# Gated linear attention before a mixture of experts: the attention output formed in 32-row array tiles, turned by VectorE instead of TensorE, and the state decay moved to ScalarE

## What is computed

```python
# q, k, v, alpha: (4, 8, 768, 48)
for t in range(S):
    state = alpha[:, :, t, :, None] * state + np.einsum('bhd,bhe->bhde', k[:, :, t], v[:, :, t])
    y[:, :, t] = np.einsum('bhd,bhde->bhe', q[:, :, t], state)
x = y.transpose(0, 2, 1, 3).reshape(3072, 384)
p = domain_probs / (domain_probs.sum(-1, keepdims=True) + 1e-09)
x2 = sum(p[:, e:e + 1] * (np.maximum(x @ w1[e], 0.0) @ w2[e]) for e in range(4))   # w1 (4, 384, 1024)
h = x2 @ w_in                                                                      # (384, 2048)
out = (h * np.clip(h + 3.0, 0.0, 6.0) / 6.0) @ w_out
```

## Time and profile before

| | |
|---|---|
| median of 3 runs | 1420.34 us (1420.33 to 1421.3) |
| the profiled execution | 1419.88 us |
| its span in the trace | 1418.1 us |
| mean granted TensorE clock | 0.996 |
| busy share PE, PEld, DVE, ACT, POOL | 98%, 80%, 52%, 38%, 59% |

### The profile page before, as it was taken

The page is one execution under the profiler, slowest core; times in us unless marked ns, Lnnn a source line. Parts: engine busy times, 40 slices in busy tenths (PEclk is TensorE's granted clock), DMA queues, the critical chain, the costliest instruction groups (busy, mean ns, idle before and its releaser), DMA issues.

```text
span 1418.1 us, 30461 instructions
## 1 busy us (share of the span) xinstructions
PE 1388.5 (98%) x11672; PEld 1140.5 (80%) x11672; DVE 731.3 (52%) x1383; ACT 533.6 (38%) x927; POOL 837.6 (59%) x870
## 2 busy tenths in 40 slices
PE   6789999999999999999999999999999999999998
PEld 5678888888888888888888888888888888888887
DVE  6977665545554555455545455555455343333343
ACT  2133333333344333344433335433334443335553
POOL 8867776565666565656665656565655444444442
PEclk9899999999999999999999999999999999999999
DMA  4333333333333433334333333443332333233330
GB/s 142 119 120 108 102 110 96 106 93 115 93 104 124 138 93 107 93 109 128 107 115 116 93 107 93 136 123 107 93 93 82 113 118 100 90 100 92 99 123 34
DMA packets 70366, 150.10 MB, mean 106 GB/s; under 512 B 9296, under 2 KB 21840, under 8 KB 70224
## 3 DMA queue, kind: packets, MB, share of 16 engines
q1 hardware_dynamic: 70224, 148.16, 34.5%
HBM read 143.36 MB, written 4.77 MB: 104 GB/s over the span
## 4 chain that ended last, share of the span: by engine, by line
PE 93%; POOL 4%; issue 1%; DVE 1%; ACT 0%; DMA 0%; DVEq 0%; POOLq 0%; ACTq 0%
PE h_bank L446 41%; PE out_banks L462 28%; PE out_third L462 14%; PE score_banks L358 4%; POOL k_lev L828 2%; PE score_banks L420 2%; PE turn_bank L398 1%; POOL decay L802 1%; PE score_banks L414 1%; PE turn_bank L386 1%; PE turn_bank L388 1%; POOL w_lo L842 1%; PE turn_bank L374 1%; POOL k_lev L818 0%; DMA alpha_q<-qa 0%
## 5 line engine op out<-in xcount | busy, mean ns | idle before, releaser
L842 POOL TENSOR_TENSOR w_lo<-w_raw,w_hi 128x768 fp32r<-128x768 f32 x288 | 547.6, 1902 | 528.2 <-ACT w_hi L745 528.0
L739 ACT ACTIVATE h_hi<-gated 128x512 fp32r<-128x512 f32 x288 | 182.2, 633 | 670.5 <-DVE gated L590 582.3
L446 PE MATMUL h_bank<-x_hi,w_hi 128*128 128x512 f32 x864 | 336.4, 389 | 1.1 <-issue 1.1
L446 PE MATMUL h_bank<-x_lo,w_hi 128*128 128x512 f32 x864 | 336.1, 389 | 0.0
L446 PE MATMUL h_bank<-x_hi,w_lo 128*128 128x512 f32 x864 | 336.0, 389 | 0.0
L590 DVE SCALAR_TENSOR_TENSOR gated<-h_bank,probs 128x512 f32<-128x512 f32 x192 | 132.7, 691 | 328.0 <-PE h_bank L446 328.0
L604 DVE TENSOR_TENSOR h_lo<-gated,h_hi 128x512 fp32r<-128x512 f32 x288 | 241.6, 839 | 57.5 <-ACT h_hi L739 57.5
L745 ACT ACTIVATE w_hi<-w_raw 128x768 fp32r<-128x768 f32 x288 | 239.1, 830 | 8.0 <-DMA w_raw<-w 8.0
L462 PE MATMUL out_banks<-h_hi,w_hi 128*128 128x512 f32 x576 | 233.0, 405 | 0.3 <-DVE x_lo L614 0.3
L462 PE MATMUL out_banks<-h_hi,w_lo 128*128 128x512 f32 x576 | 225.0, 391 | 0.0
L462 PE MATMUL out_banks<-h_lo,w_hi 128*128 128x512 f32 x576 | 224.5, 390 | 0.0
(11 more groups left out here) (75 smaller groups left out, 1279.5 us busy)
## 6 DMA issues: line engine op xcount, KB each, us to landing
w_raw<-w SPq DMA_DIRECT2D x288, 384.0 KB, 3.1
alpha_q<-qa SPq DMA_DIRECT2D x48, 256.0 KB, 3.5
k_raw<-kk SPq DMA_DIRECT2D x48, 128.0 KB, 3.5
probs<-prob_scratch SPq DMA_DIRECT2D x6, 1024.0 KB, 7.5
v_diag<-v SPq DMA_DIRECT2D x96, 48.0 KB, 2.4
out<-result SPq DMA_DIRECT2D x18, 256.0 KB, 3.9
level_sb<-level SPq DMA_DIRECT2D x1, 80.0 KB, 3.1
ident_sb<-ident SPq DMA_DIRECT2D x1, 64.0 KB, 2.8
```

The costliest lines, as they stand in the source:

```text
L446: mm = pe.matmul(h_bank[g % 2][:, :], a, x, start=k == 0 and i == 0, stop=k == K3 - 1 and i == 2)
L739: act.activation(h_hi[:, g % DEEP, :], gated[:, g % 2, :], ACT.Copy).then_inc(hh_made, 1)
L842: pool.tensor_tensor(w_lo[:, g % RING, :], w_raw[:, g % RAW, :], w_hi[:, g % RING, :].bitcast(F32), ALU.subtract).then_inc(w_lo_made, 1)
```

## The change

- `attend(n)` writes each output into a quarter of the partitions. `quarter(i, jp)` is 32 partitions, 64i+32jp. The 64 steps of a chunk are two halves `th`; half `th` is 32 columns of weights. L414 becomes 8 matmuls (16 instructions) on tiles of 128 rows by 32 columns, still 96 values moving; L420 becomes 16 matmuls (32 instructions) on tiles of 64 rows by 32 columns, 48 values moving.
- `copy_y` on ACT and `turn_y` on TensorE are gone. A new `turn_y(n)` on DVE turns 32x32 blocks straight from PSUM to SBUF (`y_turned`), two instructions of 64 partitions by 192 elements, right behind `next_state(n)`. The order of channels that comes out differs, so the host orders the rows of `w1` to match.
- `split_x` reads `y_turned` in SBUF instead of PSUM, on ACT and on DVE, one slot after the state slot. `TURN_AT` is gone. The bank (now `state_bank`) holds `kv_out` and `kt_out` alone, and the waits of `turn_k` and `carry` on `x_hi_made` and `x_lo_made` go.
- `decay_state(n)` moves from DVE (one instruction) to ACT, four instructions of 128x48 with `total` as scale, in the slot after the score slot, in the prologue after `copy_k_rows(n)`.

The core of the diff (declarations, semaphore names and the host's index arithmetic left out):

```diff
@@ tensor engine @@
             def score(n):
-                need(pe, ys_made, 2 * (n - 1) if n <= PER_TILE else 2 * n)
+                need(pe, yt_made, 2 * (n - 1) if n <= PER_TILE else 2 * n)
...
             def turn_k(n):
                 need(pe, s_made, carried(n))
-                need(pe, x_hi_made, n - 1)
-                need(pe, x_lo_made, n - 1)
-                if n % PER_TILE == 0:
-                    need(pe, x_hi_made, n)
-                    need(pe, x_lo_made, n)
...
-            def turn_y(n):
-                pe.wait_ge(ys_made, 2 * (n + 1))
-                need(pe, s_made, carried(n + 1))
-                need(pe, x_hi_made, n)
-                need(pe, x_lo_made, n)
-                rows = y_rows[n % 2]
-                for i in range(2):
-                    pe.matmul(turn_bank[own(i), P:P + CH], rows[:, P:STATE], ident_sb[:, own(i)],
-                              start=True, stop=True)
-                pe.transpose(turn_bank[:, 0:P], rows[:, 0:P], ident_sb[:, :]).then_inc(xt_made, 1)
...
             def attend(n):
-                for jp in range(2):
-                    for i in range(2):
-                        lo = 512 * i + jp * 2 * HEAD_D
-                        mm = pe.matmul(y_out[own(i), lo:lo + 2 * HEAD_D], p_kept[:, i, jp, :],
-                                       v_diag[n % 2][:, :, jp, i, :], start=jp == 0, stop=not inter,
-                                       skip_group_check=True)
-                for j in range(PAIRS if inter else 0):
-                    for i in range(2):
-                        lo = 512 * i + j * HEAD_D
-                        mm = pe.matmul(y_out[own(i), lo:lo + HEAD_D], q_level(n, LEVELS)[own(i), j, :],
-                                       state[n % 2][own(i), j, :], start=False, stop=True,
-                                       skip_group_check=True)
+                for th in range(2):
+                    for jp in range(2):
+                        for i in range(2):
+                            lo = 512 * i + th * 2 * HEAD_D
+                            mm = pe.matmul(y_out[quarter(i, jp), lo:lo + 2 * HEAD_D],
+                                           p_kept[:, i, jp, 32 * th:32 * th + 32], v_diag[n % 2][:, :, jp, i, :],
+                                           start=th == 0, stop=not inter, skip_group_check=True)
+                for th in range(2 if inter else 0):
+                    for jj in range(2):
+                        for jp in range(2):
+                            for i in range(2):
+                                j, lo = 2 * jp + jj, 512 * i + (2 * th + jj) * HEAD_D
+                                mm = pe.matmul(y_out[quarter(i, jp), lo:lo + HEAD_D],
+                                               q_level(n, LEVELS)[own(i), j, 32 * th:32 * th + 32],
+                                               state[n % 2][own(i), j, :], start=False, stop=True,
+                                               skip_group_check=True)
...
@@ vector engine @@
-            def decay_state(n):
-                dve.tensor_tensor(state_decayed[:, :, :], state[n % 2][:, :, :], ...
+            def turn_y(n):
+                dve.wait_ge(y_made, n + 1)
+                need(dve, x_hi_made, n - 1)
+                need(dve, x_lo_made, n - 1)
+                for i in range(2):
+                    dve.transpose(y_turned[n % 2][own(i), :, :].rearrange("p b (h t) -> p h b t", t=32),
+                                  scores(n)[own(i), 512 * i:512 * i + STATE].rearrange(
+                                      "p (h b e) -> p h b e", h=2, e=32)).then_inc(yt_made, 1)
...
                 if g - 1 in SCORE_AT:
-                    n = SCORE_AT[g - 1]
-                    if n % PER_TILE > 0:
-                        split_x(n - 1)
-                    keep_all(n, 3, KEEPS)
-                    if not first_of_seq(n) and not last_of_seq(n):
-                        decay_state(n)
+                    keep_all(SCORE_AT[g - 1], 3, KEEPS)
+                if g - 1 in STATE_AT:
+                    split_x(STATE_AT[g - 1])
...
+                if g in STATE_AT:
+                    n = STATE_AT[g]
+                    if not last_of_seq(n):
+                        next_state(n)
+                    turn_y(n)
@@ scalar engine @@
-            def copy_y(n):
-                for i in range(2):
-                    act.activation(y_rows[n % 2][own(i), :], scores(n)[own(i), 512 * i:512 * i + STATE], ACT.Copy
+            def decay_state(n):
+                act.wait_ge(s_made, carried(n))
+                act.wait_ge(z_made, Z_STEPS * (n + 1))
+                for j in range(PAIRS):
+                    act.activation(state_decayed[:, j, :], state[n % 2][:, j, :], ACT.Copy,
+                                   scale=total[n % 2][:, j:j + 1]).then_inc(dec_made, 1)
```

More of the change, by code:

```diff
@@ L86 @@
 STATE_AT = {state_slot(n): n for n in range(PER_TILE, CHUNKS)}
-TURN_AT = {score_slot(n) + (4 if n < 2 * PER_TILE else 5): n for n in range(2 * PER_TILE - 1, CHUNKS, PER_TILE)}
 def spread(share):
@@ L476, in _ @@
                 keep_warm(2)
-                turn_y(n)
                 if n + 1 < PER_TILE:
@@ L577, in split_x @@
                 dve.wait_ge(x_hi_made, n + 1)
-                if (n + 1) % PER_TILE and not last_of_seq(n + 1):
-                    dve.wait_ge(kn_made, carried(n + 1) + 1)
-                dve.tensor_tensor(x_lo[:, r, :, cols], kv_out.rearrange("p (k t) -> p k t", t=CH),
+                dve.tensor_tensor(x_lo[:, r, :, cols], y_turned[n % 2][:, :, :],
                                   x_hi[:, r, :, cols].bitcast(F32), ALU.subtract).then_inc(x_lo_made, 1)
@@ L671, in _ @@
                 if g - 1 in SCORE_AT:
-                    n = SCORE_AT[g - 1]
-                    if n % PER_TILE > 0:
-                        split_x(n - 1)
-                    keep_all(n, 3, KEEPS)
-                    if not first_of_seq(n) and not last_of_seq(n):
-                        decay_state(n)
+                    keep_all(SCORE_AT[g - 1], 3, KEEPS)
+                if g - 1 in STATE_AT:
+                    split_x(STATE_AT[g - 1])
                 if g in SCORE_AT:
                     keep_all(SCORE_AT[g], 0, 3)
-                if g in STATE_AT and not last_of_seq(STATE_AT[g]):
-                    next_state(STATE_AT[g])
-                if g in TURN_AT:
-                    split_x(TURN_AT[g])
+                if g in STATE_AT:
+                    n = STATE_AT[g]
+                    if not last_of_seq(n):
+                        next_state(n)
+                    turn_y(n)
                 if g in Q_AT:
@@ L759, in _ @@
             for n in range(PER_TILE):
-                if n > 0:
-                    split_x(n - 1)
                 copy_k_rows(n)
+                if not first_of_seq(n):
+                    decay_state(n)
                 odd_k(n + 2)
-                copy_y(n)
-            split_x(PER_TILE - 1)
+                split_x(n)
             for g in range(SLOTS):
@@ L779, in _ @@
                         odd_k(n + 2)
-                if g in STATE_AT:
-                    copy_y(STATE_AT[g])
-                if g in TURN_AT:
-                    split_x(TURN_AT[g])
+                if g - 1 in SCORE_AT:
+                    n = SCORE_AT[g - 1]
+                    if not first_of_seq(n) and not last_of_seq(n):
+                        decay_state(n)
+                if g - 1 in STATE_AT:
+                    split_x(STATE_AT[g - 1])
                 if g >= BEHIND and g - BEHIND + 1 in STARTS and PHASES[PHASE_OF[g - BEHIND]][0] == "E":
@@ L899 @@
     dm, ft = H * D, 8
-    f = np.arange(pairs * D)
-    row = [(2 * (f // D) + i) * D + f % D for i in range(2)]
-    order = np.concatenate([row[0][:P], row[1][:P], row[0][P:], row[1][P:]])
+    b, i, jp, f = np.ix_(range(dm // P), range(2), range(2), range(32))
+    jj, e = np.divmod(32 * b + f, D)
+    order = ((2 * (2 * jp + jj) + i) * D + e).reshape(-1)
     def pack(w1, w2):
```

40 lines of the change are left out of this document (11 added, 29 removed).

## The result

Before 1420.34 us (13 runs), after **1423.28 us** (1421.24 to 1425.02, 13 runs): ratio 1.002, 95% interval 1.0011 to 1.0028. The forecast was 1405.0 us in 1398 to 1415. The change costs 2 to 4 us; it was to give 15.

A forecast was written before the change was run, and what follows sets the result against it. Past the prologue TensorE's own order of work bounds the kernel, in the prologue DVE. Terms -16.1 + 3.6 - 1.3 - 1.5 = -15.3 us take 1420.34 to 1405.0 us, range 1398 to 1415.

The forecast's parts named there:

- The step that failed: DVE, main part: two transposes add 0.6 us, L557's 0.35 goes per chunk, `split_x` moves earlier; no cost.
- The prologue: DVE's rounds lose 0.90 us of decay and gain 0.6 of transposes; six rounds give -1.5 us, bounds -3 and +10.
- DVE paces it, with POOL just behind: Prologue: DVE's rounds follow every 7.17 us without idle time; POOL waits 0.29 us in each for `decay_state`.
- turns: Turn matmuls leave TensorE: 13.3 us from 35 score slots and 2.8 from 5 turn-only slots, together -16.1 us.
- the wait in slot 3: `score(9)` waits for DVE's earlier `turn_y(8)` instead of ACT's copy: -1.3 us, 0 if DVE is as late.
- The narrower tiles: TensorE's `attend`: L414 stays 0.33 us, L420 falls to 0.55, one more shape change costs 0.15; +3.6 us, bounds -6 and +6.
- TensorE waiting for DVE at `score`: A sign in the profile after that would show the prediction wrong; no size given.
- ACT: Gains four 128x48 decays, at most 1.3 us, and loses two L713 of 0.32: net 0.65 per chunk, fits its idle time.
- Narrow tiles that do not overlap: Rival in `attend`: L414 takes 0.66 us and L420 1.07, +36 us in all, giving 1437 us; chance 0.07.
- starts as the floor: Rival in `attend`: 48 starts at 23 ns each take 1.12 us, so no change, 1420 us; chance 0.04.
- Transposes of 1.0 us: Rival on DVE: slow transposes make the prologue cost 8.8 us instead of -1.5, giving 1415 us; chance 0.07.
- idle time of PE behind slot 0: Main part: the profile after was to show none of it; no size given.

The follow-up runs named there:

- experiment 2: Changed kernel with DVE's `split_x` one slot later in the main part, two slots behind the state slot, ACT's unmoved: 1407.71 us, ratio 0.9911 to the kernel before.
- 6: On the kernel with DVE's later `split_x`: prologue `turn_y` moved to the end of DVE's round, behind the last `scale_q` steps; 1409.0 us, ratio 0.9921.
- 9: On the kernel with DVE's later `split_x`: the prologue's `x_lo` subtraction of chunks 0 to 5 on POOL instead of DVE; 1407.48 us, ratio 0.9911.
- 3: Changed kernel with `decay_state` back on DVE as one instruction, in prologue and main part, nothing on ACT: 1426.01 us, ratio 1.0035 to the kernel before.
- 1: Changed kernel with ACT's prologue `odd_k(n+2)` moved ahead of `copy_k_rows(n)` and `decay_state(n)`: 1424.86 us, ratio 1.0034 to the kernel before.
- 7: On the kernel with DVE's later `split_x`: ACT's prologue `odd_k` one chunk further ahead; 1410.32 us, ratio 0.9931.
- 8: On the kernel with DVE's later `split_x`: six idle matmuls instead of two at three `keep_warm` places per prologue chunk; 1407.95 us, ratio 0.9917.
- 11: On the kernel with DVE's later `split_x`: prologue forms one `x_lo` column and turns one 32x32 block in place of six; 1404.81 us, one execution.
- 12: On the kernel with DVE's later `split_x`: prologue forms one `x_lo` column per chunk, all block transposes done; 1409.46 us, one execution.

## Why the prediction was wrong

**The step that failed** is "In the main part DVE adds 0.6 and loses L557's some 0.35 per chunk, beside 328 us of waiting for TensorE: no cost", with "`split_x` moves from the next score slot to the slot behind the state slot". It saw that the result would be ready early and took early for harmless. It named what is queued behind `turn_y`, and never did so for `split_x`. Moved there, DVE stood for 1.7 to 2.2 us for an `x_hi` that ACT makes later in the same slot, with `keep` and the next `hidden_lo` behind it. And that the second operand went from PSUM to SBUF was not costed: 0.35 became 1.61 us, since POOL's `w_lo` runs at that moment. The idle 328 us were a sum over the span; in nine slots, five of them in tile 1, there was no slack for it. Undone by one slot of delay, 14.0 us came back (experiment 2).

**The prologue** was to give 1.5 us and cost 6.2 (5.3 in experiment 2). The step: "A round loses `decay_state`, 44.92 - 44.02 = 0.90 us, and gains 0.6: -0.3 us". One round of DVE after, the one that answers to the earlier trace rows:

```profile
42.34 0.43 DVE L521 TENSOR_TENSOR p_kept<-out_banks,diag_sb 128x256 f32<-128x256 f32 x1
42.80 1.78 DVE L532 COPY_PREDICATED p_kept<-level_sb,out_banks 128x128 f32<-128x128 int32 x5
44.47 0.82 DVE L562 TENSOR_TENSOR x_lo<-y_turned,x_hi 128x192 fp32r<-128x192 f32 x1
45.21 0.28 DVE L497 TENSOR_TENSOR alpha_q<-alpha_q 128x128 f32<-128x128 f32 x1
...
46.99 0.78 DVE L554 STREAM_TRANSPOSE y_turned<-out_banks 64x192 f32<-64x192 f32 x2
47.81 2.12 DVE L508 TENSOR_TENSOR q_lev<-q_lev,decay 128x256 f32<-128x256 f32 x4
49.96 0.42 DVE L521 TENSOR_TENSOR p_kept<-score_banks,diag_sb 128x256 f32<-128x256 f32 x1
```

It is 49.96 - 42.34 = 7.62 us instead of 7.17. The turn takes 47.81 - 46.99 = 0.82 where 0.6 was taken, nearly the 0.90 that the decay gave back, and `x_lo` 45.21 - 44.47 = 0.74, where it took 0.27 before (42.15 to the next start, 42.42): a cost that the round did not count. In experiment 2 DVE's busy time up to the first hidden is 67.23 us, 2.25 more than before. The rest is waiting, most of it for TensorE:

```profile
55.60 0.79 DVE L554 STREAM_TRANSPOSE y_turned<-score_banks 64x192 f32<-64x192 f32 x2 [1.11 <-PE score_banks L407]
...
75.35 0.79 DVE L554 STREAM_TRANSPOSE y_turned<-score_banks 64x192 f32<-64x192 f32 x2 [1.20 <-PE score_banks L407]
```

With 0.46 and 0.31 elsewhere in it these are 3.1 us, so 2.25 + 3.1 = 5.3: DVE now waits in its round for the `attend` of the same chunk. That is where DVE's time went, not a proof of what set the length: busy and idle time of any engine add up to the stretch, and POOL's idle time grew by 6.5 us. No edit gained by one term alone: without the waits DVE grew busier (6), and with the subtraction on POOL POOL did (9). What is shown is that in DVE's round the turn and the subtraction cost more than the decay gave back, that the decay on ACT is worth 2 to 3 us (3), and that earlier copies on ACT and a higher clock in the prologue bring nothing (1, 7, 8). The transposes cost something (11 against 12). How the prologue's 5 to 6 us divide stays open.

The chain of work shows a pace that the prediction had otherwise. Followed back from the first L446, the chain of the kernel before is POOL for 58.7 of the 80.7 us and DVE for 3.3: POOL's decays and key scaling come round every 7.17 us too, with 0.26 us between two rounds. "DVE paces it, with POOL just behind" does not fit that; DVE counted by the 0.29 us in which POOL waited for it. In experiment 2 the same chain, from 38 us on, is POOL for 18.8 us, TensorE 11.2, DVE 7.4 and ACT 2.7. Part of it in order of time:

```profile
49.47 2.35 PE out_banks L361 x92
...
55.53 1.15 PE h_bank L415 x4
...
57.38 1.00 ACT state_decayed L692 x4
```

So TensorE's scores and `keep_warm` matmuls, at a granted clock of 0.66 from 50.5 to 60 us, and ACT's four decays now stand in the way of POOL. Taking away one link (7, 8) gained nothing either, as another took its place; no run takes them all.

**The sum, term by term.** Measured against forecast: turns -0.1, `attend` -3.7, the wait in slot 3 +0.35, the prologue +7.7 (6.2 + 1.5), and new stalls +13.9 where the sum had nothing. That is 18.1 us, and the spans are 2.7 + 15.3 = 18.0 us from the forecast. Nothing in the total came out by luck: the errors that helped, 3.8 us, are small beside the 21.6 us of the two that failed.

**What held.** The turns: -16.1 forecast, -16.2 measured; the score slots are like the earlier trace rows and no turn is left. The narrower tiles: +3.6 forecast, -0.1 measured (by its own terms the bounds were -6.7 and +6.4, not -6 and +6). The p group grew by 0.14 us (0.15 taken for the change of shape), but L407 fell to 0.47, not 0.55: 32 starts of 14.7 ns. The wait in slot 3: -1.3 forecast, -0.95 measured, 0.33 us are left, for DVE's turn; TensorE waiting for DVE at `score` had been named as a sign of being wrong:

```profile
101.27 0.43 PE L361 MATMUL score_banks<-alpha_q,k_raw 64*64 64x32 f32 x16 [0.33 <-DVE y_turned L554]
```

ACT: the four decays take 0.32 us each as bounded, and late was not ACT but the place at which DVE asked it.

```profile
L692 ACT ACTIVATE state_decayed<-state,total 128x48 f32<-128x48 f32 x160 | 39.9, 320 | 0.0
```

**The rivals.** Narrow tiles that do not overlap (1437) and starts as the floor (1420) both asked for `attend` to grow by 0.47 us per chunk; it grew by 0.006. That the time is near the second is chance. The estimate from the Trainium skill, TensorEngine Tiling (Array Packing), "Instruction Overhead", 60 cycles or 25 ns for every start and so 1.2 us for 48, is not borne out: 48 starts and two changes of shape took 0.94 us. Transposes of 1.0 us (1415) took 0.379. None of the rivals was a wait on another engine in the main part, though the idle time of PE behind slot 0 was named as a sign; the sign came. The range failed with it: its upper end held the prologue's bounds and nothing for a new wait.

## What to carry to other kernels

An engine that idles a quarter of the time can still be late in one slot. When a step is moved earlier, look up in which order its inputs are made in that very slot, and put the reader a slot behind the maker. When an operand moves from PSUM to SBUF, count the instruction's SBUF inputs and look which GpSimd instructions run beside it: its price can become the length of theirs. To compare two prologues, take the first point behind which the traces are alike, look at the granted clock there, and take more than one execution.

## What the runs showed that was not expected

- A DVE subtraction with two SBUF inputs beside POOL's 128x768: one every 1.88 us instead of 0.39, at 128x192, and POOL not slowed; on one column in the prologue still 0.35 us on the mean. One PSUM input, or a block transpose: no difference.
- A 64x192 block transpose from PSUM takes 0.374 us alone, about what a 128x192 subtraction takes.
- Four column tiles of 32 under 128 rows: 16 instructions that move 96 values in 0.47 us with the change of shape, 8 on two tiles in 0.48 with it (L399 and L382 above).
- The same matmuls of slot 0 took 3.98 us or up to 6.73 us, by the granted clock in it: 1.00 or 0.54 (experiments 2 and 9).
